# Opening, first value products and first ReLU tiles of a fused attention, expert and dense kernel, set in another order

## The reference

```python
q_assign = np.argmax(np.einsum('bhsd,hcd->bhsc', q_n, c_n), axis=-1)
k_assign = np.argmax(np.einsum('bhsd,hcd->bhsc', k_n, c_n), axis=-1)
mask = q_assign[:, :, :, None] == k_assign[:, :, None, :]
scores = np.where(mask, scale * np.matmul(q, k.transpose(0, 1, 3, 2)), -1000000000.0)
attn = softmax(scores);  x = attn @ v                      # (1536, 512)
expert_idx = np.argmax(x @ w_gate, axis=1)                 # 8 experts
out[mask] = gate_w[mask, None] * (np.maximum(xe @ w1[e], 0.0) @ w2[e])
h = x @ w_in                                               # (1536, 2048)
return (np.maximum(h, 0.0) + alpha * np.minimum(h, 0.0)) @ w_out
```

## Time and profile before

| | us |
|---|---|
| median of 3 runs | 821.28 |
| lowest, highest | 819.19, 822.26 |
| profiled execution | 820.07 |
| its span | 818.2 |
| TensorE busy | 783.4 |
| VectorE busy | 387.6 |
| ScalarE busy | 296.8 |

### The profile page before, as it was taken

One profiled execution on the slowest core, in us unless ns is written; L12 is line 12 of the kernel. 1 busy time (PEld: TensorE's weight loads), 2 busy tenths in 40 slices (PEclk: granted clock), 3 DMA queues, 4 the chain that ended last, 5 costly groups with the idle time before them and its releaser, 6 DMA issues.

```text
span 818.2 us, 13290 instructions
## 1 busy us (share of the span) xinstructions
PE 783.4 (96%) x5289; PEld 728.5 (89%) x5289; DVE 387.6 (47%) x629; ACT 296.8 (36%) x446; POOL 162.1 (20%) x153
## 2 busy tenths in 40 slices
PE   4889999999999999699999999989999999999996
PEld 4789999999999999699999999988888888888885
DVE  5634454444545446956665555555451413322230
ACT  2434343333433532345555555543222201211011
POOL 3312113121231003540000000005042412323141
PEclk9889999999999999999999999999999999999999
DMA  5646556465674715667666555505001000000001
GB/s 127 137 96 148 134 132 150 103 148 129 136 202 112 206 34 172 196 141 231 228 229 220 195 192 185 202 12 195 1 0 39 14 1 0 26 26 0 1 14 38
DMA packets 76028, 93.13 MB, mean 114 GB/s; under 512 B 45968, under 2 KB 45968, under 8 KB 75984
## 3 DMA queue, kind: packets, MB, share of 16 engines
q1 hardware_dynamic: 73680, 86.20, 38.2%
q0 software_dynamic: 2304, 6.31, 2.0%
HBM read 59.31 MB, written 12.73 MB: 88 GB/s over the span
## 4 chain that ended last, share of the span: by engine, by line
PE 59%; DVE 2%; ACT 0%; issue 0%; POOL 0%; ACTq 0%; DVEq 0%
PE psS L1260 5%; PE psS L1261 5%; PE psS L1259 5%; PE psVD L1210 4%; PE psVD L1209 4%; PE psVD L1208 4%; PE psS L1192 4%; PE psS L1193 4%; PE psS L1194 4%; PE psVD L1278 3%; PE psM L1278 3%; PE psVD L1276 3%; PE psVD L1277 3%; PE psM L1276 3%; PE psM L1277 3%; PE psM L1171 1%
## 5 line engine op out<-in xcount | busy, mean ns | idle before, releaser
L639 PE MATMUL psVD<-Vp,PT 128*128 128x128 f32 x1152 | 148.5, 276 | 0.0
L639 PEld LDWEIGHTS psVD<-Vp,PT 128*128 128x128 f32 x1152 | 144.6, 192 | 0.6
L1646 POOL TENSOR_TENSOR g_lo<-gf,g_hi 128x512 fp32r<-128x512 f32 x48 | 62.1, 1294 | 329.0 <-ACT g_hi L1400 328.8
L930 DVE TENSOR_REDUCE neg_max<-psM 128x1 f32<-128x768 f32 x90 | 86.2, 958 | 73.8 <-PE psM L613 73.8
L480 DVE TENSOR_TENSOR w_lo<-w_raw,w_hi 128x1024 fp32r<-128x1024 f32 x88 | 105.0, 1223 | 23.8 <-ACT w_hi L476 23.8
L793 ACT ACTIVATE PT<-psS 128x768 f32<-128x768 f32 x96 | 76.4, 811 | 87.7 <-PE psS L631 87.7
L1603 DVE TENSOR_SCALAR tmin<-psS,alpha_c 128x512 f32<-128x512 f32 x48 | 36.0, 751 | 148.2 <-PE psS L1261 148.1
L476 ACT ACTIVATE w_hi<-w_raw 128x1024 fp32r<-128x1024 f32 x88 | 90.3, 1056 | 0.9 <-DMA w_raw<-in_moe_w 0.9
L1400 ACT ACTIVATE g_hi<-gf 128x512 fp32r<-128x512 f32 x48 | 30.3, 632 | 161.9 <-DVE gf L1606 161.9
L1192 PE MATMUL psS<-xe_hi,w_hi 128*128 128x224 f32 x288 | 80.4, 279 | 6.0 <-DVE ht_lo L1530 4.5
L1193 PE MATMUL psS<-xe_lo,w_hi 128*128 128x224 f32 x288 | 80.4, 279 | 0.0
(11 more groups left out here) (226 smaller groups left out, 1424.4 us busy)
## 6 DMA issues: line engine op xcount, KB each, us to landing
w_raw<-in_moe_w SPq DMA_DIRECT2D x18, 2048.0 KB, 8.9
xs_slots<-zero SPq DMA_DIRECT2D x8, 784.0 KB
K<-Kh SPq DMA_DIRECT2D x32, 192.0 KB, 2.8
w_raw<-in_moe_w_in SPq DMA_DIRECT2D x2, 2048.0 KB, 8.1
w_raw<-in_moe_w_out SPq DMA_DIRECT2D x2, 2048.0 KB, 11.1
xe_n<-xs_slots SPq DMA_DIRECT2D x16, 224.0 KB, 8.6
Qn<-in_q SPq DMA_DIRECT2D x16, 192.0 KB, 4.1
Kn<-in_k SPq DMA_DIRECT2D x16, 192.0 KB, 4.2
```

The lines of the kernel that those rows point to most:

```text
L639: mm = pe.matmul(psV[:, PVS * t:PVS * t + P], PT[par][:, c, t * P:(t + 1) * P], Vp[par][:, c, :], start=(c == 0), stop=(c == T - 1))
```

## The change

Six things, on all engines.

1. **Opening, loads and fills.** The centroids are loaded first, then both queries, then both keys; `s_qk` becomes `s_qn` and `s_kn`, so that query transposes wait for queries alone. VectorE's memsets come in another order; those of `warm`, `settle`, `wg` and the scan pads go to GpSimd, those of the ones rows of `K2` behind the `lo` tiles.
2. **Fillers.** `keep_warm(n)` multiplies the identity with itself into `psS` bank 3, whose result nobody reads: 10 ahead of the first transposes, 8 ahead of the one-hot transposes, 2 ahead of the first maximum tile, 3 before and 3 after the first `max_row`.
3. **Opening, one-hots.** The dots of the queries go to `psD`, those of the keys to `psV`, and `onehots_first` makes the five steps for the queries and then for the keys. ScalarE makes the first `Qh`, `Kh`, VectorE the first `Kl`, `Ql` (in this order, behind the one-hots), and GpSimd none of them. SyncE's first four copies wait for `Kl` alone.
4. **Value products.** Halves 0 to 5 of head 0 move from slot 1 into slot 0, two each at three places behind its last maximum tile. The first two wait for all of head 1's maxima.
5. **Item 0.** The ReLU tiles 0 to 3 have memory of their own (`first_hi`, `first_lo`, in rows 2 and 3 of `Y`), so ScalarE waits for the scatters only ahead of tile 4. VectorE makes `lo` tiles between the weight quarters; `late_items` is split into `items_found` and `positions` with tiles 4 to 7 between them; the item loop leaves out what is done ahead of it. The first output copy waits for `s_pos`. The last gather is split so that ScalarE can start after half of it, and tile 0 multiplies `xe_hi` with both weight parts before it needs `xe_lo`. GpSimd issues scatters 6 to 11 ahead of reading `early_i`; a new `s_slotted` stands beside `s_scat`.
6. **Dense layer.** The first tile of `widen` multiplies all of `y_hi` before `y_lo`.

```diff
             def load_qk(j):
                 for par in range(2):
-                    sp.dma_start(Qn[:, :, par * D:(par + 1) * D], qd[2 * j + par]).then_inc(s_qk, 16)
-                    sp.dma_start(Kn[:, :, par * D:(par + 1) * D], kd[2 * j + par]).then_inc(s_qk, 16)
+                    sp.dma_start(Qn[:, :, par * D:(par + 1) * D], qd[2 * j + par]).then_inc(s_qn, 16)
+                for par in range(2):
+                    sp.dma_start(Kn[:, :, par * D:(par + 1) * D], kd[2 * j + par]).then_inc(s_kn, 16)
...
+            sp.dma_start(cent[:, :], centroids.rearrange("h c d -> (h c) d")).then_inc(s_cent, 16)
             load_qk(0)
-            sp.dma_start(cent[:, :], centroids.rearrange("h c d -> (h c) d")).then_inc(s_cent, 16)
...
             sp.wait_ge(s_hi, 2)
-            sp.wait_ge(s_lo, 2)
+            sp.wait_ge(s_lo, 1)
             assemble_parts(0)
             sp.wait_ge(s_oh, 1)
+            sp.wait_ge(s_lo, 2)
             assemble_rest(0)
...
+            def keep_warm(n):
+                for _ in range(n):
+                    pe.matmul(psS[:, 3, 0:P], ident[:, :], ident[:, :], start=True, stop=True)
+
+            pe.wait_ge(s_const, 1)
+            keep_warm(WARM0)
+            pe.wait_ge(s_qn, 32)
             transpose_raw(Qn)
...
+            pe.wait_ge(s_kn, 32)
+            transpose_raw(Kn, psS, 0)
             pe.wait_ge(s_cbd, 2)
-            dots(0, 0)
-
+            dots(0, 0, range(T), done=s_dot0)
+            dots(0, 0, range(T, 2 * T), ps=psV)
+            keep_warm(WARM1)
             transpose_onehots(0)
...
-                    if t > 0 and prev:
+                    if t > 0 and prev and not second:
                         output(t - 1)
-                if prev:
+                if prev and not second:
                     output(T - 1)
                 if after:
                     maximum(T - 1)
+                if not prev:
+                    pe.wait_ge(s_v[0], 16)
+                    pe.wait_ge(s_exp, T)
+                    pe.wait_ge(s_nm, 2 * T)
+                    out_half(0, 0)
+                    out_half(0, 1)
...
                 if not odd and nxt:
                     pe.wait_ge(s_nm, T * (g + 2))
                     transpose_onehots(j + 1)
+                if not prev:
+                    out_half(0, 2)
+                    out_half(0, 3)
...
             dve.wait_ge(s_const, 2)
-            hi_parts(0, True)
-            for n in range(5):
-                onehot_step(0, n, True)
+            for i in range(2):
+                onehots_first(i)
+            dve.wait_ge(s_hi, 2)
+            for lo, full, hi in ((Kl, KTr, Kh), (Ql, QTr, Qh)):
+                nc.vector.tensor_tensor(lo[:, :], full[:, :], hi[:, :].bitcast(F32),
+                                        ALU.subtract).then_inc(s_lo, 1)
...
+        def hidden_at(first, f):
+            if first and f < FT1 // 2:
+                return first_hi[:, f, :], first_lo[:, f, :]
+            return ht_hi[:, f, :], ht_lo[:, f, :]
...
-            for c in range(4):
-                hi_quarter(1, c, s_whi)
+            hi_quarter(1, 0, s_whi)
+            hi_quarter(1, 1, s_whi)
+            hidden_hi(0, 0, True)
+            hi_quarter(1, 2, s_whi)
+            hidden_hi(0, 1, True)
+            hi_quarter(1, 3, s_whi)
+            hidden_hi(0, 2, True)
+            act.wait_ge(s_rw[0], 32)
+            hidden_hi(0, 3, True)
             act.wait_ge(s_scat, 16 * NT)
+            act.wait_ge(s_slotted, 1)
+            for f in range(FT1 // 2, FT1):
+                hidden_hi(0, f, True)
+                hi_quarter(2, f - FT1 // 2, s_whi)
...
             xe_lo_part(0)
-            late_items()
             for c in range(4):
                 dve.wait_ge(s_whi, 4 + c + 1)
                 lo_quarter(nc.vector, 1, c, s_wlo)
+                hidden_lo(0, c, True)
+            items_found()
+            for f in range(FT1 // 2, FT1):
+                hidden_lo(0, f, True)
+            positions()
+            for c in range(4):
+                dve.wait_ge(s_whi, 8 + c + 1)
+                lo_quarter(nc.vector, 2, c, s_wlo)
...
             pool.wait_ge(s_slot, 1)
+            for u in range(T, NT):
+                scatter(u, slot_u, s_scat)
             early_over = pool.value_load(early_i[0:1, 0:1], min_val=0, max_val=NE)
```

More of the change, by code:

```diff
@@ L44 @@
 PVS = 66
+WARM0, WARM1, WARM2, WARM3 = 10, 8, 2, 3
 QK1 = 112
@@ L1325, in body @@
                         at = item_place(act, it)
-                    for f in range(FT1):
+                    for f in range(0 if not (first and par == 0) else FT1, FT1):
                         hidden_hi(it, f)
```

176 lines of the change are left out of this document (131 added, 45 removed).

## The result

| | kernel before | kernel changed |
|---|---|---|
| median of four runs | 821.63 us (819.19 to 822.26) | 813.51 us (811.74 to 813.93) |
| ratio to before | | 0.9902, 95% interval 0.9885 to 0.9919 |
| profiled execution, its span | 820.07, 818.2 us | 813.93, 812.1 us |
| mean granted clock | 0.982 | 0.992 |

The kernel is 8.1 us faster by the medians and 6.1 us by the two profiled spans. I had forecast 806.5, with a range of 803 to 812: the direction was right, the size was not, and the time lies above the range.

The account below looks back on a forecast made before the run. TensorE, busy 96% of the span, was taken as the bound, with time in opening, item 0 and dense entry: -6.8 - 6.4 - 0.8 = -14.0 on 820.07 gives 806.1; forecast 806.5 us, range 803 to 812.

Parts of the forecast that it names:

- opening, to slot 2: Opening with slots 0 and 1: slot 2 starts at 60.15 instead of 66.95, -6.8 us (-2.3 to -7.8).
- item 0: First expert item: the 4.5 us wait for `ht_lo` goes, item 1 starts at 359.1 instead of 365.57; -6.4 us.
- item 1 to the dense block, with its entry: Entry to the dense block: first tile starts on `y_hi` at 544.35 instead of waiting for `y_lo` until 545.18; -0.8 us.
- dense block: Dense products behind the entry: TensorE runs without a wait at 2.4 GHz and nothing there is changed; 0 us.
- Opening, first part: Up to the first maximum tile: it starts at 20.3 instead of 22.58 us, a gain of 2.25 us.
- Slots 0 and 1: First two slots: slot 0 begins at 28.6, slot 1 at 41.95, slot 2 at 60.15 instead of 66.95 us.
- Slot 1 starts at ... 41.95: End of slot 0: from VectorE's last reduction at 36.95, value halves, one-hot transposes and copies bring slot 1 at 41.95 us.
- rival A: Ahead of the first maximum tile TensorE idles about 1.7 us, the clock falls, slot 0 slows: 809.5 us; chance 15%.
- new fillers stand in exactly the later gaps: Argument against the clock falling in the opening: the later gaps have fillers; no size of its own.
- The moved value products: Six halves moved to slot 0: one pair, 1.3 us, on its path; slot 1 loses 3.9 us of TensorE work.
- Rivals B and C: Position scatters collide with weight loads: B 808 to 811 us, chance 11%; C 823 and more, chance 3%.
- the -2.4: Entry to the dense block: the gain if the shorter gap also spares the fall of the clock.

Follow-up runs that it names:

- no_fill: Changed kernel with the kernel before's addresses restored (new 32-byte tile behind the weights) and all its 26 fillers left out; ratio to the kernel before 0.9886.
- warm_all: Changed kernel with new 32-byte tile behind the weights, twelve fillers added in slots 0 and 1, seven more ahead of the first maximum tile; 809.90 us, ratio 0.9845.
- best: Changed kernel with addresses of before, nineteen added fillers, and item 1's `xe_hi` and `xe_lo` ahead of the last weight quarters; 806.55 us, ratio to before 0.9823.
- best2: best with head 0's value products back in slot 1, 4, 4 and 3 fillers in slot 0's last waits, none in slot 1; 806.48 us, ratio 0.9778.
- item_only: Kernel before with only item 0's part of the change, at the addresses of before; 816.16 us, ratio to before 0.9905.
- after_again: Changed kernel run once more without any edit; profiled span 817.1 us.
- layout: Changed kernel with its new 32-byte tile moved behind weights and activations, giving these the kernel before's addresses; ratio to before 0.9875.
- layout_r5: The changed kernel with the kernel before's addresses (layout), timed once more in another group; 811.83 us, ratio to before 0.9842.

## Why the prediction failed, step by step

| term | forecast | profiled pair |
|---|---|---|
| opening, to slot 2 | -6.8 | -2.4 |
| item 0 (profiled: slot 2 to item 1) | -6.4 | -6.5 |
| item 1 to the dense block, with its entry | -0.8 | -0.7 |
| dense block | 0 | +3.5 |
| sum | -14.0 | -6.1 |

**Opening, first part: right.** First maximum tile at 20.61 (20.3 said), slot 0 at 28.90 (28.6). The keys were there by 7.24, earlier than the 7.8 taken (the 1.3 us at 7.16 that the prediction gives for them were those of the queries; the keys followed at the same pace), and half steps on one-hots ended at 13.7 (13.9). That transposes run at half the time once the clock is up was right, against the rule of the Trainium skill that I had weighed (page "TensorE: Matmul & The Clock Gate", section "Part 4: PE-mode transpose"): the six of the keys took 0.85 us at 7.24 and later ones 0.82 to 0.87, against 1.51 at the lower clock (no_fill). Whether transposes alone bring the clock up no run shows, since other products stand between them.

**Slots 0 and 1: the failed step is "Slot 1 starts at ... 41.95".** It takes the full clock over a place where the same paragraph puts a new wait on TensorE, behind a maximum tile that waits too. The engine did 0.80 us of work in 2 us there, and 0.89 in 2 us was what I had seen ahead of a fall. What it overlooked stood in the trace of before, where the clock fell at the end of slot 0 (from about 44) behind waits of the same kind. I had put the danger ahead of the first maximum tile (rival A, 15%), and the argument "new fillers stand in exactly the later gaps" was false for these gaps: they had none. In all nine other profiles with the change's own two fillers ahead of the first maximum tile, the clock fell at rival A's place as well. Two falls at 1.6 us make 3.3 of the missing 4.4; slot 1's period of 1.67 us instead of 1.62 and a slower first slot make the rest. At the full clock (warm_all) slot 2 starts at 61.47, 1.3 above the 60.15. Rival A was the right mechanism at too low a chance, and in the five profiles of the changed kernel, at either address, it strikes two or three times ahead of slot 2.

**The moved value products: right size in slot 0 (1.3 said, 1.5 found), wrong in slot 1.** The forecast made slot 1 18.2 us long instead of the 21.2 before (45.76 to 66.95), as if moving the products shortened it. It does not: at the full clock it takes 18.6 us with them moved (best) and 18.7 without (best2), and the 21.2 held a fall of the clock (44 to 51). By these two profiles that part of the change costs about 1.4 us.

**Item 0: right.** 6.0 of the 6.5 us lie between `xe_hi` and item 1 (31.1 us before, 25.1 changed), 0.5 ahead of it. Layer 1 ended at 343.20 (345.65 less the 2.96 us by which the item started earlier: 342.7), item 1 started at 356.62 (by the same count 356.1), behind a wait of 1.76 us for `xe_lo` (1.9). Rivals B and C did not occur: between 356 and 535 us TensorE waits for nothing, and ScalarE never for a weight load. item_only confirms it alone (25.20). The wait for `xe_lo` can cost the clock too, as after_again and layout show; the forecast put nothing for that.

**Entry: right.** 0.66 of 0.8; the clock fell in spite of the shorter gap, so the -2.4 was not had.

**Dense block: the step that was not there.** The forecast says "elsewhere TensorE runs without a wait at 2.4 GHz, and nothing there is changed". The instructions were not changed, the addresses were, by 32 bytes. This is 3.5 us of the miss. With the addresses of before the ratios (0.9842 in layout_r5, 0.9875 in layout) give 809 to 811 us, which is within the range of 803 to 812, but that would have been luck in part: by the medians the opening gave 5.3 of its 6.8 us and item 0 8.7 instead of 6.4, and the second surplus, which the forecast doesn't have, makes up for the first gap.

## What to carry to other kernels

A gain that frees time on TensorE is only had if the waits it leaves don't cost the clock: look at every stretch in which the change adds a wait, not only where the old kernel lost the clock, and put fillers there first. A new tile belongs behind the tiles of the hot loops; when a kernel gets slower in a place that was not touched, compare the mean time of the same instructions there, and then the addresses. Work moved into an earlier wait pays only if it can start before that wait ends: here the moved products stood behind the last reduction, on which the chain to the next slot hangs as well. And before a mend is credited with a time, compare its kernel with the one it is measured against line by line: warm_all's 5.3 us hold 3 to 3.5 for the addresses.
